# Moving a fused kernel's weights and matmul operands to 512-byte boundaries of the on-chip memory

## The chip, the cores and the metric

The kernel runs on one core of a Trainium2 chip. The metric is the device time of one execution in microseconds (us). Times of the kernel before come from three runs; the rows further down come from one profiled execution.

## What is computed

Three stages, one after the other, all in float32 (reference cut to its core):

```python
X = fft(fft(x, axis=1), axis=2).real                 # x: 4 x 3072 x 256
xk = mu_k * X + (1 - mu_k) * X_prev                  # X_prev: X moved by one token
xr = mu_r * X + (1 - mu_r) * X_prev
k = maximum(xk @ w_k, 0)                             # 256 x 1024
x3 = sigmoid(xr @ w_r) * ((k * k) @ w_v)             # 256 x 256, 1024 x 256
# a mixture of 8 experts over the 12288 rows of x3: expert = argmax of x3 @ w_gate,
# each expert takes its first 384 rows, in order of the tokens
h = maximum(rows_of_expert @ w1[e], 0)
out[row] = probability * (h @ w2[e])                 # rows that no expert took stay 0
```

## The kernel before

The program is written out by engine, with a semaphore for each hand-over; nothing in it orders work by cost, and every address in the on-chip memory is fixed when it is built.

The Fourier transform of a batch is three steps of small matmuls (step1, L1301; step2, L1316; step3, L1328). The middle stage then goes over tiles of 512 tokens (TOK), six to a batch. For a tile, VectorE forms the two mixes (`difference`, `mix`), ScalarE and VectorE split each mix into a high part and a low part (`xk[:, 0]`, `xk[:, 1]`, and `xr` alike), and TensorE multiplies. Every float32 product is made of three matmuls in the faster float32 format (fp32r): high x high, high x low, low x high (`product`, L303). A tile has 8 `up` products of 6 matmuls (weights `wk`, moving operand `xk`), 8 `down` steps of 6 (weights `wv`, moving `k2`) and 12 matmuls for the gate (weights `wr`, moving `xr`). All of them move 512 columns, except 16 of the very first tile that move halves of 256 (`opening_ups`, L1434). Between `up` and `down` stand, for each f, ScalarE's relu (L776) and its copy of the square's high part (L771), and VectorE's square (L1102) and low part (L1097). The Fourier steps of the next batch are put between the products of tiles 3 to 5 of a batch.

After each tile its rows are routed to the experts. When all eight are full, which with these inputs is after 14 tiles, every engine leaves the loop. The expert stage uses other buffers: `xe` (moving, 384 columns, weights `up0_high`, `up0_low`, `up1`) and `down_w` (moving, 256 columns, weights `he`), again three fp32r matmuls to a product.

Addresses: `sb(...)` reserves a buffer of the on-chip memory. The buffers lie one behind the other in the order of the calls, each at the next multiple of 32 bytes (of the bytes of one partition, the same in all 128). A buffer in a `with ExitStack()` of its own gives its place back, so that the next one lies over it: `k2` lies over `raw_wk`, `raw_wr`, `first_partner`, `between` and `raw_wv`. `ph(...)` (L141) reserves what only the Fourier and the middle stage use; `phase1.close()` (L433) gives all of it back, and the expert stage's buffers begin at the same place.

From the sizes in the code: the first `ph` buffer begins at byte 54,784, which is 107 x 512. Then come `c_first` with 6,760 bytes, `c_second` with 1,032 and `c_third` with 960. They and their padding take 8,800 bytes, or 17 x 512 + 96, so `wk`, `wv` and `wr` all begin 96 bytes past a multiple of 512. Behind `wr` come buffers of odd sizes up to `xt`, and `xr_raw`, `xk_raw`, `xk`, `xr`, `relu`, `square`, the `k2` group, `gate_r` and `x3` all begin 224 bytes past one. Both remainders are multiples of 32 and not of 64. In the expert stage `xe`, `raw_up_0`, `raw_up_1`, `raw_down1`, `up1`, `down_w0`, `down_w1` and `he` begin at multiples of 512, and so do `up0_low` and `up0_high`.

Of the kernel before, what the change touches and what calls it, by code (L numbers as in the profile page):

```python
# [18 lines left out]
P = 128  # L19
BATCH, SEQ, DIM, FF = 4, 3072, 256, 1024  # L20
# [5 lines left out]
SETS = FOLDED + 1  # L26
# [14 lines left out]
DH = DIM // P  # L41
FT = FF // P
TOK = 512
# [9 lines left out]
K2S = 8  # L53
# [42 lines left out]
def build(nc, ins, out, cap):  # L96
    fp32, bf16, fp32r = mybir.dt.float32, mybir.dt.bfloat16, mybir.dt.float32r
# [13 lines left out]
    def sb(name, shape, dt=fp32, where=ctx):  # L111
        return where.enter_context(nc.sbuf_tensor(name, shape, dt))
# [26 lines left out]


    ph = lambda name, shape, dt=fp32: sb(name, shape, dt, phase1)  # L141
    c_first = ph("c_first_sb", [P, NR, 2 * JOWN])
    c_second = ph("c_second_sb", [P, ZW])
    c_third = ph("c_third_sb", [P, C3_COLS])
    m_even, m_odd = c_third[0:ROWS2, 0:SCOLS], c_third[0:ROWS2, SCOLS:2 * SCOLS]

    wk = ph("wk", [P, 2, DH, FF], fp32r)
    wv = ph("wv", [P, 2, FT, DIM], fp32r)
    wr = ph("wr", [P, 2, DH, DIM], fp32r)
    fan = ph("fan", [P, DH, SPLIT])  # L150
    mu_k = ph("mu_k", [P, DH])
    mu_r = ph("mu_r", [P, DH])
# [8 lines left out]
    odd_copy = ph("odd_copy", [P, 2, 4 * SCOLS])  # L161
    later_partner = y[:, :, :, :].rearrange("p o q r -> p (o q r)")[:, 0:SETS * DIM].rearrange("p (a d) -> p a d", a=SETS)
    xt = ph("xt", [P, DH, SEQ + 2])
    xr_raw = ph("xr_raw", [P, DH, TOK])
    xk_raw = ph("xk_raw", [P, DH, TOK])
    xk = ph("xk", [P, 2, DH, TOK], fp32r)
    xr = ph("xr", [P, 2, DH, TOK], fp32r)

    relu = ph("relu", [P, 2, TOK])
    square = ph("square", [P, 2, TOK])  # L170
    with ExitStack() as before_k2:
        raw_wk = sb("raw_wk", [P, DH, FF], fp32, before_k2)
        raw_wr = sb("raw_wr", [P, DH, DIM], fp32, before_k2)
        first_partner = sb("first_partner", [P, SETS, DIM], fp32, before_k2)
        sb("between", [P, 2 * K2S * TOK - DH * FF - DH * DIM - FT * DIM - SETS * DIM], fp32, before_k2)
        raw_wv = sb("raw_wv", [P, FT, DIM], fp32, before_k2)
    k2 = ph("k2", [P, 2, K2S, TOK], fp32r)
    gate_r = ph("gate_r", [P, DH, TOK])
    x3 = ph("x3", [P, DH, TOK])
    blank = ph("blank", [P, ROW])  # L180
    least = ph("least", [P, NTILE + 2], i32)
    base = ph("base", [P, EXPERTS])
# [1502 lines left out]
```

## Time and profile before

| | |
|---|---|
| median of 3 runs | 606.15 us (605.74 to 606.67) |
| the profiled execution's own time | 605.92 us |
| its span, first to last instruction | 604.1 us |
| TensorE (PE) busy | 592.7 us, 98% |
| weight loads (PEld) busy | 512.9 us, 85% |
| VectorE (DVE) busy | 449.2 us, 74% |
| ScalarE (ACT) busy | 319.7 us, 53% |
| GpSimd (POOL) busy | 97.5 us, 16% |

How to read it: matmuls run in a pipeline, so that one is still under way when the next begins. The duration of one (some 396 ns for 512 columns) is therefore not what it costs in a dense row of them. What it costs is the time from one start to the next, which is the start of a run of matmuls taken from the start of what follows it, divided by their count. Or the busy time of a run less the duration of its last matmul, divided by one less than their count.

### The profile page before, as it was taken

How to read it: one execution, taken by the hardware profiler on the slowest of the kernel's cores; microseconds unless marked ns; L12 is line 12 of the kernel's file. 1: busy time of each engine (PE TensorE's matmuls, PEld its weight loads, DVE VectorE, ACT ScalarE, POOL GpSimd, SP SyncE). 2: the span in 40 equal slices, each digit the busy share in tenths (PEclk: the TensorE clock that was granted, in tenths of full speed). 3: DMA queues.
4: the chain of work that ended last, by engine and by line, in shares of the span. 5: the costliest groups of instructions: out<-in, count | busy, mean ns of one | idle time of the engine just before them, and what ended most of it. 6: DMA issues, size and time to landing. Idle time of an engine off the chain costs nothing.

```text
span 604.1 us, 9905 instructions
## 1 busy us (share of the span) xinstructions
PE 592.7 (98%) x3356; PEld 512.9 (85%) x3356; DVE 449.2 (74%) x1046; ACT 319.7 (53%) x731; POOL 97.5 (16%) x101
## 2 busy tenths in 40 slices
PE   8999999999999999999999999999998999999996
PEld 4978788888888888888888888888887999999996
DVE  4688888877777688888777776688886777766672
ACT  1674645554546564645454536564647555664450
POOL 0710302020202010202020202011202111011111
PEclk9999999999999999999999999999999999999999
DMA  9429936241510005201010100024003944455100
GB/s 310 153 73 215 395 138 204 94 142 53 185 52 24 2 11 187 105 0 57 10 38 1 34 1 5 30 67 173 32 0 105 365 158 135 160 194 179 41 28 27
DMA packets 42168, 63.14 MB, mean 105 GB/s; under 512 B 4582, under 2 KB 32055, under 8 KB 42108
## 3 DMA queue, kind: packets, MB, share of 16 engines
q1 hardware_dynamic: 38268, 55.88, 28.5%
q0 software_dynamic: 3840, 6.52, 3.1%
q8 instruction: 30, 0.49, 0.3%
q14 instruction: 30, 0.25, 0.1%
HBM read 39.90 MB, written 26.91 MB: 111 GB/s over the span
## 4 chain that ended last, share of the span: by engine, by line
PE 93%; DVE 1%; ACT 1%; SPq 1%; DMA 1%; issue 1%; POOLq 0%; ACTq 0%; DVEq 0%
PE bank L303 71%; PE bank L1407 6%; PE bank L1372 4%; PE bank L1316 3%; PE bank L1328 2%; PE bank L1301 2%; DMA first_partner<-in_x 1%; PE bank L1599 1%; PE bank L1420 1%; DVE xt L958 0%; SPq L485 0%; SPq L496 0%; PE bank L1608 0%; PE bank L1609 0%; PE bank L1612 0%
## 5 line engine op out<-in xcount | busy, mean ns | idle before, releaser
L303 PE MATMUL bank<-k,wv 128*128 128x512 f32 x672 | 165.3, 396 | 0.0
L303 PEld LDWEIGHTS bank<-k,wv 128*128 128x128 f32 x672 | 125.7, 188 | 28.8
L303 PE MATMUL bank<-xk,wk 128*128 128x512 f32 x492 | 124.0, 398 | 0.0
L645 POOL DMA_INDIRECT dispatched<-rows,slot x56 | 60.8, 1086 | 361.2 <-DVE slot L1073 348.4
L303 PEld LDWEIGHTS bank<-xk,wk 128*128 128x128 f32 x492 | 91.3, 189 | 20.0
L776 ACT ACTIVATE relu<-bank 128x512 f32<-128x512 f32 x114 | 67.8, 598 | 74.6 <-PE bank L303 63.1
L1102 DVE TENSOR_TENSOR square<-relu 128x512 f32<-128x512 f32 x113 | 77.9, 691 | 35.0 <-ACT relu L776 31.5
L1097 DVE TENSOR_TENSOR k<-square,k 128x512 fp32r<-128x512 f32 x112 | 76.9, 687 | 2.8 <-ACT k L771 2.8
L771 ACT ACTIVATE k<-square 128x512 fp32r<-128x512 f32 x113 | 70.7, 626 | 11.5 <-DVE square L1102 11.4
L303 PE MATMUL bank<-down_w,he 128*128 128x256 f32 x576 | 72.0, 284 | 0.0
L303 PEld LDWEIGHTS bank<-down_w,he 128*128 128x128 f32 x576 | 70.4, 191 | 0.0
L1267 DVE SCALAR_TENSOR_TENSOR he<-bank,he 128x384 fp32r<-128x384 f32 x64 | 35.7, 558 | 35.3 <-ACT he L898 34.9
L898 ACT ACTIVATE he<-bank 128x384 fp32r<-128x384 f32 x64 | 31.5, 492 | 55.8 <-PE bank L303 29.3
L665 POOL DMA_INDIRECT out_rows<-ye,who x24 | 23.4, 973 | 116.4 <-DVE ye L1281 95.4
L1407 PE MATMUL bank<-xk,wk 128*128 128x512 f32 x144 | 41.2, 409 | 0.0
L303 PE MATMUL bank<-xr,wr 128*128 128x512 f32 x162 | 40.1, 396 | 0.0
L303 PEld LDWEIGHTS bank<-xr,wr 128*128 128x128 f32 x162 | 30.4, 188 | 6.9
L1116 DVE TENSOR_TENSOR x<-gate_r,bank 128x512 f32<-128x512 f32 x28 | 19.1, 687 | 18.6 <-PE bank L303 18.5
L757 ACT ACTIVATE rows<-bank 128x16 f32<-128x16 f32 x56 | 9.5, 184 | 42.6 <-PE bank L1372 41.4
L751 ACT ACTIVATE xr<-xr_raw 128x512 fp32r<-128x512 f32 x30 | 19.0, 633 | 24.4 <-DVE xr_raw L969 24.0
L303 PE MATMUL bank<-xe,up_high 128*128 128x384 f32 x112 | 28.5, 335 | 1.6 <-DVE he L1267 1.6
L303 PE MATMUL bank<-xe,up 128*128 128x384 f32 x168 | 29.8, 334 | 0.0
(151 smaller groups left out, 796.4 us busy)
## 6 DMA issues: line engine op xcount, KB each, us to landing
out_rows<-blank SPq DMA_DIRECT2D x16, 768.0 KB, 4.5
raw_up<-in_moe_w SPq DMA_DIRECT2D x8, 1024.0 KB, 5.2
raw_down<-in_moe_w SPq DMA_DIRECT2D x8, 1024.0 KB, 9.0
got<-dispatched SPq DMA_DIRECT2D x16, 409.5 KB, 3.0
x_area<-in_x SPq DMA_DIRECT2D x12, 384.0 KB, 5.8
y<-in_x SPq DMA_DIRECT2D x9, 384.0 KB, 7.7
dispatched<-blank SPq DMA_DIRECT2D x1, 3276.0 KB, 19.6
first_partner<-in_x SPq DMA_DIRECT2D x3, 384.0 KB, 6.3
```

Of the source, the lines that this page charges most:

```text
L303: done = nc.tensor.matmul(bank, w, x, start=first and i == 0, stop=last and i == len(terms) - 1)
L645: nc.gpsimd.indirect_dma_start(out=slots_dram, out_offset=bass.IndirectOffsetOnAxis(ap=slot[:, g:g + 1], axis=0), in_=rows[:, g, :], in_of ...
L665: nc.gpsimd.indirect_dma_start(out=out, out_offset=bass.IndirectOffsetOnAxis(ap=who[:, i, j:j + 1], axis=0), in_=ye[:, i, j, :], in_offset ...
L771: nc.scalar.activation(k2_at(0, f), square[:, f % 2, :], ACT.Copy).then_inc(k2_high, 1)
L776: nc.scalar.activation(relu[:, f % 2, :], up_bank(n, f)[:, :], ACT.Relu).then_inc(hb_drained, 1)
L898: nc.scalar.activation(he[:, 0, f, :], hbe[f % 3][:, 0:cap], ACT.Relu).then_inc(he_high, 1)
L1097: nc.vector.tensor_tensor(k2_at(1, f), square[:, f % 2, :], k2_at(0, f).bitcast(fp32), ALU.subtract).then_inc(squared, 1)
L1102: nc.vector.tensor_tensor(square[:, f % 2, :], relu[:, f % 2, :], relu[:, f % 2, :], ALU.mult).then_inc(square_ready, 1)
L1116: nc.vector.tensor_tensor(x3[:, h, :], gate_r[:, h, :], vb[h][:, :], ALU.mult).then_inc(x3_done, 1)
L1267: nc.vector.scalar_tensor_tensor(he[:, 1, f, :], hbe[f % 3][:, 0:cap], 0.0, he[:, 0, f, :].bitcast(fp32), ALU.max, ALU.subtract).then_inc( ...
L1372: done = mm(tb[g][:, h * SPLIT:(h + 1) * SPLIT], x3[:, h, g * P:(g + 1) * P], fan[:, h, :], start=True, stop=True)
L1407: done = mm(hb[f % 2][:, :], *terms[k], start=k == 0, stop=k == len(terms) - 1)
```

## The change

The order of the calls to `ph` is changed, and nothing else. `wk`, `wv`, `wr`, `xr_raw`, `xk_raw`, `xk`, `xr`, `relu`, `square`, the group under `k2`, `k2`, `gate_r` and `x3` are reserved first. Their sizes are all multiples of 512 bytes, so each begins at a multiple of 512. `c_first`, `c_second`, `c_third` and the other buffers follow. The moved buffers take 110,592 bytes together, or 216 x 512, which is how far the three constants move up; everything from `fan` to `xt` moves up by 73,728, or 144 x 512. So these keep their remainders by 512. From `blank` on, and in the expert stage, every address is what it was. No instruction, wait, transfer or size changes.

```diff
     ph = lambda name, shape, dt=fp32: sb(name, shape, dt, phase1)
+    wk = ph("wk", [P, 2, DH, FF], fp32r)
+    wv = ph("wv", [P, 2, FT, DIM], fp32r)
+    wr = ph("wr", [P, 2, DH, DIM], fp32r)
+    xr_raw = ph("xr_raw", [P, DH, TOK])
+    xk_raw = ph("xk_raw", [P, DH, TOK])
+    xk = ph("xk", [P, 2, DH, TOK], fp32r)
+    xr = ph("xr", [P, 2, DH, TOK], fp32r)
+    relu = ph("relu", [P, 2, TOK])
+    square = ph("square", [P, 2, TOK])
+    with ExitStack() as before_k2:
+        raw_wk = sb("raw_wk", [P, DH, FF], fp32, before_k2)
+        raw_wr = sb("raw_wr", [P, DH, DIM], fp32, before_k2)
+        first_partner = sb("first_partner", [P, SETS, DIM], fp32, before_k2)
+        sb("between", [P, 2 * K2S * TOK - DH * FF - DH * DIM - FT * DIM - SETS * DIM], fp32, before_k2)
+        raw_wv = sb("raw_wv", [P, FT, DIM], fp32, before_k2)
+    k2 = ph("k2", [P, 2, K2S, TOK], fp32r)
+    gate_r = ph("gate_r", [P, DH, TOK])
+    x3 = ph("x3", [P, DH, TOK])
+
     c_first = ph("c_first_sb", [P, NR, 2 * JOWN])
     c_second = ph("c_second_sb", [P, ZW])
     c_third = ph("c_third_sb", [P, C3_COLS])
     m_even, m_odd = c_third[0:ROWS2, 0:SCOLS], c_third[0:ROWS2, SCOLS:2 * SCOLS]
 
-    wk = ph("wk", [P, 2, DH, FF], fp32r)
-    wv = ph("wv", [P, 2, FT, DIM], fp32r)
-    wr = ph("wr", [P, 2, DH, DIM], fp32r)
     fan = ph("fan", [P, DH, SPLIT])
...
     xt = ph("xt", [P, DH, SEQ + 2])
-    xr_raw = ph("xr_raw", [P, DH, TOK])
...
-    x3 = ph("x3", [P, DH, TOK])
     blank = ph("blank", [P, ROW])
```

## Rows read from the trace of the kernel before

**Rows 1.** The page, busy time and share of the span of each engine.
```profile
PE 592.7 (98%) x3356; PEld 512.9 (85%) x3356; DVE 449.2 (74%) x1046; ACT 319.7 (53%) x731; POOL 97.5 (16%) x101
```
**Rows 2.** Stretch, busy PE, PEld, DVE, ACT, POOL, granted clock, DMA share, GB/s.
```profile
44.00:100.00 56.00, 56.00 (x267) 45.79 (x266) 46.52 (x102) 31.18 (x65) 9.20 (x8) 1.00 0.83 245
100.00:250.00 150.00, 149.74 (x792) 124.78 (x791) 115.14 (x267) 79.91 (x172) 19.32 (x18) 1.00 0.26 89
400.00:455.00 55.00, 55.00 (x266) 44.89 (x265) 44.92 (x109) 29.36 (x64) 8.52 (x8) 1.00 0.22 75
```
**Rows 3.** Whom TensorE waited for, the longest: us in total, times, longest.
```profile
PE bank L385 <- DVE relu L910: 2.0, 1, 2.0
```
**Rows 4.** TensorE's groups, shapes kept apart: count, busy us, mean ns.
```profile
L303 PE MATMUL bank<-k,wv 128*128 128x512 f32 x672 | 165.3, 396 | 0.0
L303 PE MATMUL bank<-xk,wk 128*128 128x512 f32 x492 | 124.0, 398 | 0.0
L1407 PE MATMUL bank<-xk,wk 128*128 128x512 f32 x144 | 41.2, 409 | 0.0
```
**Rows 5.** Timeline of TensorE, middle stage: start us, busy us, what.
```profile
103.84 8.53 PE L303 MATMUL bank<-k,wv 128*128 128x512 f32 x36
112.20 0.63 PE L1407 MATMUL bank<-xk,wk 128*128 128x512 f32 x2
```
**Rows 6.** The critical chain in order of time, two of its pieces.
```profile
8.17 6.61 DMA first_partner<-in_x
62.87 22.31 PE bank L303 x96
```
**Rows 7.** Timeline of TensorE, expert stage.
```profile
512.61 7.44 PE L303 MATMUL bank<-xe,up 128*128 128x384 f32 x42
519.88 3.03 PE L303 MATMUL bank<-down_w,he 128*128 128x256 f32 x24
523.76 5.55 PE L303 MATMUL bank<-down_w,he 128*128 128x256 f32 x45
```
**Rows 8.** Timeline of TensorE, 33.5 to 34.2 us: nine of the opening's half-width matmuls.
```profile
33.22 1.23 PE L1434 MATMUL bank<-xk,wk 128*128 128x256 f32 x9
```
**Rows 9.** Single matmuls by tile: duration ns min/median/max, first and last start.
```profile
L303 PE MATMUL bank<-k,wv x672: 387/393/496, 43.8 to 449.1; 128*128 128x512 f32 x168
L303 PE MATMUL bank<-xe,up x168: 333/334/335, 477.4 to 590.1; 128*128 128x384 f32 x168
L1434 PE MATMUL bank<-xk,wk x16: 279/282/361, 32.5 to 34.4; 128*128 128x256 f32 x16
L303 PE MATMUL bank<-down_w,he x576: 278/283/364, 467.1 to 598.8; 128*128 128x256 f32 x192
```
**Rows 10.** VectorE's and ScalarE's groups: count, busy us, mean ns.
```profile
L1102 DVE TENSOR_TENSOR square<-relu 128x512 f32<-128x512 f32 x113 | 77.9, 691 | 35.0 <-ACT relu L776 31.5
L1267 DVE SCALAR_TENSOR_TENSOR he<-bank,he 128x384 fp32r<-128x384 f32 x64 | 35.7, 558 | 35.3 <-ACT he L898 34.9
L1246 DVE TENSOR_TENSOR down_w<-raw_down,down_w 128x256 fp32r<-128x256 f32 x56 | 19.4, 422 | 0.0
L771 ACT ACTIVATE k<-square 128x512 fp32r<-128x512 f32 x113 | 70.7, 626 | 11.5 <-DVE square L1102 11.4
L885 ACT ACTIVATE down_w<-raw_down 128x256 fp32r<-128x256 f32 x56 | 17.9, 413 | 1.0 <-DMA raw_down<-in_moe_w 1.0
L808 ACT ACTIVATE gate_r<-bank 128x512 f32<-128x512 f32 x28 | 16.6, 598 | 13.6 <-PE bank L303 13.5
L898 ACT ACTIVATE he<-bank 128x384 fp32r<-128x384 f32 x64 | 31.5, 492 | 55.8 <-PE bank L303 29.3 <-PE bank L1612 25.9 <-issue 0.7
```
**Rows 11.** The page, DMA issues: KB each, median us from issue to landing.
```profile
y<-in_x SPq DMA_DIRECT2D x9, 384.0 KB, 7.7
x_area<-in_x SPq DMA_DIRECT2D x12, 384.0 KB, 5.8
first_partner<-in_x SPq DMA_DIRECT2D x3, 384.0 KB, 6.3
```

More of the change, by code:

```diff
@@ L141, in build @@
     ph = lambda name, shape, dt=fp32: sb(name, shape, dt, phase1)
[L142 to L145, printed above, removed]
     wk = ph("wk", [P, 2, DH, FF], fp32r)
@@ L149, in build @@
     wr = ph("wr", [P, 2, DH, DIM], fp32r)
-    fan = ph("fan", [P, DH, SPLIT])
-    mu_k = ph("mu_k", [P, DH])
-    mu_r = ph("mu_r", [P, DH])
-    earlier = ph("earlier", [P, P], bf16)
-    ones = ph("ones", [P, P], bf16)
-    x_area = ph("x_area", [P, max(SETS * DIM, SG * ZW)])
-    x_own = x_area[:, 0:SETS * DIM].rearrange("p (a d) -> p a d", a=SETS)
-    apart = ph("apart", [P, 2])
-    z = x_area[0:ROWS2, 0:SG * ZW].rearrange("p (q k) -> p q k", q=SG)
-    edge = ph("edge", [N2, N1])
-    far_copy = ph("far_copy", [P, 2, 6 * JOWN])
-    odd_copy = ph("odd_copy", [P, 2, 4 * SCOLS])
-    later_partner = y[:, :, :, :].rearrange("p o q r -> p (o q r)")[:, 0:SETS * DIM].rearrange("p (a d) -> p a d", a=SETS)
-    xt = ph("xt", [P, DH, SEQ + 2])
     xr_raw = ph("xr_raw", [P, DH, TOK])
@@ L179, in build @@
     x3 = ph("x3", [P, DH, TOK])
+    c_first = ph("c_first_sb", [P, NR, 2 * JOWN])
+    c_second = ph("c_second_sb", [P, ZW])
+    c_third = ph("c_third_sb", [P, C3_COLS])
+    m_even, m_odd = c_third[0:ROWS2, 0:SCOLS], c_third[0:ROWS2, SCOLS:2 * SCOLS]
+    fan = ph("fan", [P, DH, SPLIT])
+    mu_k = ph("mu_k", [P, DH])
+    mu_r = ph("mu_r", [P, DH])
+    earlier = ph("earlier", [P, P], bf16)
+    ones = ph("ones", [P, P], bf16)
+    x_area = ph("x_area", [P, max(SETS * DIM, SG * ZW)])
+    x_own = x_area[:, 0:SETS * DIM].rearrange("p (a d) -> p a d", a=SETS)
+    apart = ph("apart", [P, 2])
+    z = x_area[0:ROWS2, 0:SG * ZW].rearrange("p (q k) -> p q k", q=SG)
+    edge = ph("edge", [N2, N1])
+    far_copy = ph("far_copy", [P, 2, 6 * JOWN])
+    odd_copy = ph("odd_copy", [P, 2, 4 * SCOLS])
+    later_partner = y[:, :, :, :].rearrange("p o q r -> p (o q r)")[:, 0:SETS * DIM].rearrange("p (a d) -> p a d", a=SETS)
+    xt = ph("xt", [P, DH, SEQ + 2])
     blank = ph("blank", [P, ROW])
```

## The prediction

> **What bounds the kernel now.** I read the engines' busy time first [rows 1]. TensorE is busy 98% of the span, VectorE 74%, so if an address changes anything it has to change TensorE to matter. Then the stretches [rows 2]: through the middle stage TensorE is busy without a gap (56.00 of 56.00 us, 149.74 of 150.00, 55.00 of 55.00), at the full granted clock, that is 2.4 GHz or 0.417 ns for a column. VectorE has 83% there (46.52 of 56.00), 77% (115.14 of 150.00) and 82% (44.92 of 55.00). TensorE's longest wait on anyone in the whole span is 2.0 us, once, at the start [rows 3]. So a matmul of the middle stage that takes less time gives nearly all of it to the end, and one that takes more costs all of it.
>
> The quantity that decides is the time from one matmul's start to the next one's. Three widths of fp32r matmul are there, each with its own remainder of the address by 512:
>
> - 512 columns, middle stage, weights 96 and moving operand 224 bytes past a boundary: 36 matmuls from 103.84 to 112.20 us, or 8.36 / 36 = 232.2 ns [rows 5]. A second stretch: 96 in 22.31 us, or 232.4 ns [rows 6]. I take 232.3.
> - 384 columns, expert stage, everything at multiples of 512: 42 from 512.61 to 519.88 us, 7.27 / 42 = 173.1 ns; by the busy time, (7.44 - 0.334) / 41 = 173.3 ns [rows 7, 9]. I take 173.3.
> - 256 columns, expert stage, at multiples of 512: (5.55 - 0.283) / 44 = 119.7 ns [rows 7, 9].
> - 256 columns, the opening of the first tile, off the boundary as the 512-wide ones are: (1.23 - 0.282) / 8 = 118.5 ns [rows 8, 9].
>
> **The change part by part.** It removes, adds and moves no instruction; only addresses differ. There are four kinds of operation whose address changes.
>
> *Fp32r matmuls of 512 columns.* Their number: 672 + 492 + 144 in the three largest groups [rows 4] and 214 in eight smaller ones, 1,522 in all. The code gives the same: 14 tiles of 48 + 48 + 12, less the 8 that the opening moves as 16 halves, and 18 of a fifteenth tile that are issued ahead of leaving the loop. Their cost at a boundary is not in the trace, so it is bounded from the aligned rows. Lower end: from 256 to 384 columns the aligned start-to-start time grows by 173.3 - 119.7 = 53.6 ns, and 128 columns at 0.417 ns are 53.3. So in the aligned stage width costs the clock alone and all else is constant (173.3 - 384 x 0.417 = 13.3 ns). One more step of 128 columns gives 173.3 + 53.3 = 226.6 ns, where the row shows 232.3: the unaligned matmul has 5.7 ns that the aligned rule doesn't explain. Upper end, if the 13.3 ns grow with width: 173.3 x 512 / 384 = 231.1 ns, 1.2 below today. Both start from the same nearest row, and nothing in the trace puts the truth nearer to either, so I take the middle, 228.85 ns, 3.45 ns less than now. 1,522 x 3.45 ns = 5.25 us, and the ends are 1,522 x 1.2 = 1.8 us and 1,522 x 5.7 = 8.7 us.
>
> A second sign that the address does something: the durations of the single aligned matmuls of 384 columns agree to 2 ns (333/334/335). Those of the 512-wide ones have 393 for a median but mean 396 [rows 4, 9], and the minimum is 387.
>
> *VectorE and ScalarE on the moved buffers.* VectorE takes 422 ns for 256 columns and 558 for 384, both on the boundary, and 691 for 512 off it: the step that crosses over costs 133 ns, the one that stays costs 136. ScalarE: from 256 columns on the boundary to 512 off it (source in the same memory, 413 and 626 ns) are 213 ns, and from 384 on to 512 off it (source in the accumulation banks, 492 and 598 ns) are 106 [rows 10]. With a rate r a column and a cost c of being off, 256 r + c = 213 and 128 r + c = 106, so that c is -1 ns. I take 0. Even 10 ns on each of the some 500 large operations of VectorE would lie under TensorE's busy time, since VectorE has 17% to spare; were that cover gone, it would cost 5 us.
>
> *Small matmuls* (Fourier steps, routing): `c_first`, `c_second`, `c_third`, `x_area`, `fan` and `y` keep their remainders. Only `x3` as weights moves. 0, within 0.2 us.
>
> *Transfers.* `first_partner`, `raw_wk`, `raw_wr` and `raw_wv` now land on boundaries. One matters: 6.61 us of `first_partner` stand in the chain that ends last [rows 6]. Transfers of 384 KB took 5.8 us into `x_area`, 6.3 into `first_partner` (both 224 past a boundary) and 7.7 into `y` (480 past one) [rows 11], so their spread is the queue's, not the address's. I take 0, bounds -0.4 and +0.4 us.
>
> The sum: 605.92 us is the profiled execution's own time (span 604.1 and 1.8 around it). 605.92 - 5.25 = 600.7. That execution lies 0.23 us under the median of the runs, which puts the forecast at 600.9 us. As TensorE gets 1.5% faster VectorE's share there goes from 83% to 84%; no new bound arises, though the places where VectorE is the later one give back a little, perhaps 0.1 us: 601.0.
>
> **The rivals.**
>
> *The address changes nothing that can be measured* (606.15 us; within 0.2%, or 1.2 us, about what a measurement can tell from no change). For it: the one width seen on and off the boundary, 256 columns, doesn't gain on it (119.7 against 118.5 ns). The 5.7 ns may then belong to the width of 512 itself, the only one here that fills a whole accumulation bank. Against it: it leaves an increment of 53.3 ns per 128 columns up to 384 and 59 behind it unexplained but by that. The Trainium skill speaks for this rival: "SBUF — State Buffer", in the note on cachelines under "Door 1: The DMA port swizzle", has lines of 16 bytes as the only grain that an engine's reads feel. All the old remainders are multiples of 32, so by that rule every operand already starts on a line, and the sum would be 605.9.
>
> *On the boundary the matmuls settle into a slower beat* (slower than before). The aligned rows are 119.7 and 173.3 ns, near 18 and 26 times 6.67 ns, with hardly any scatter, while the unaligned 256-wide ones came out at 118.5, between steps. If start times on the boundary lock to such steps, 512 columns may lock at 34 (226.7 ns, the lower end above), but also at 35, which is 233.3 ns. The price of the latter is 1.0 ns x 1,522 = 1.5 us, 607.7 us; the 256-wide pair shows the same sign and size (119.7 - 118.5 = 1.2 ns, 1.8 us if it held for all). At 36 steps, 240 ns, it would be 7.7 ns x 1,522 = 11.7 us, 617.9. It decides against the change from a start-to-start time of 233.1 ns on, where the loss passes 1.2 us. Against it: three steps over the 32 of the columns, where both aligned rows have two.
>
> *The lower end holds in full*: 605.92 - 8.7 + 0.23 = 597.5 us. It is part of the forecast's own range.
>
> **How the numbers follow.** The forecast, faster, the matmuls of 512 columns between 226.6 and 231.1 ns: 0.47, own range 597.2 to 604.6. No change: 0.35. A slower beat at 35 steps: 0.14; at 36 or worse: 0.04. The range goes from 597.0, where the lower end of the matmuls meets 0.4 us from the transfers, to 608.2, which takes in the 35 steps with the same 0.4. It leaves out the 36 steps and a gain beyond the aligned rule. Faster by over 0.2% is the forecast's 0.47, within it 0.35, slower 0.18.
>
> **What would show it.** In the timeline of the changed kernel the run of 36 matmuls of `k` and `wv` after 100 us: 228.85 ns each is 8.24 us to the next start where 8.36 stood; 8.16 is the lower end, 8.40 the slower beat. The widths of 384 and 256 in the expert stage must stay at 173.3 and 119.7, since their addresses don't move; if they change, the cause isn't the address. VectorE's 691 and ScalarE's 598 ns must stay. If TensorE's busy time in the middle stage falls below its full share, VectorE has become a bound and part of the gain is lost. The opening's nine half-width matmuls tell on or off the boundary at one width: toward 119.7 ns the address acts on them. The prediction is wrong if 512 columns keep 232.3 ns, or if they slow down.

## The result: 1.1% faster, and the middle stage's matmuls start every 226.7 ns

The changed kernel takes 599.12 us (median, 598.74 to 600.78) against 605.97 us for the kernel before in the same comparison: a ratio of 0.9888, 95% interval 0.9874 to 0.9902. Its profiled execution took 599.07 us with a span of 597.2, 6.9 us less than the 604.1 of before. The forecast was 601.0 us, within 597.0 to 608.2.

The page of the changed kernel, busy time by engine and then the two largest groups of matmuls (count, busy us, mean ns):

```profile
PE 585.8 (98%) x3356; PEld 511.7 (86%) x3356; DVE 448.8 (75%) x1046; ACT 319.4 (53%) x731; POOL 96.6 (16%) x101
...
L303 PE MATMUL bank<-k,wv 128*128 128x512 f32 x672 | 162.0, 391 | 0.0
...
L303 PE MATMUL bank<-xk,wk 128*128 128x512 f32 x492 | 121.6, 393 | 0.0
```

TensorE's busy time fell by 592.7 - 585.8 = 6.9 us [rows 1], the whole gain. Of it 165.3 - 162.0 = 3.3 us are the 672 matmuls of `k2` and `wv`, and 124.0 - 121.6 = 2.4 us the 492 of `xk` and `wk` [rows 4]. Some 0.2 us have nothing to do with the change: they are the plain float32 matmuls at the opening (L385), both of whose operands lie in `relu`, so that their distance did not change. They went from 9.5 to 9.3 us, and among the experiments they take anything from 9.0 to 10.6. VectorE's 448.8 us and ScalarE's 319.4 are within 0.4 us of what they were.

The timeline of TensorE in the changed kernel (start us, busy us, what), the run of 36 that stands in [rows 5], and the expert stage as in [rows 7]:

```profile
102.28 8.32 PE L303 MATMUL bank<-k,wv 128*128 128x512 f32 x36
110.44 0.62 PE L1407 MATMUL bank<-xk,wk 128*128 128x512 f32 x2
...
505.75 7.44 PE L303 MATMUL bank<-xe,up 128*128 128x384 f32 x42
513.03 3.03 PE L303 MATMUL bank<-down_w,he 128*128 128x256 f32 x24
```

From 102.28 to 110.44 are 8.16 us for 36, or 226.7 ns from start to start where 232.2 stood. The expert stage, whose addresses did not move, has the same 7.44 and 3.03 us as before. The waits of TensorE name nobody new, and the middle stage is still full: busy 56.00 of 56.00 us from 44 to 100, at a granted clock of 1.00, with VectorE's share at 85% where it was 83% [rows 2]:

```profile
44.00:100.00 56.00, 56.00 (x271) 46.55 (x270) 47.59 (x103) 31.20 (x66) 8.99 (x8) 1.00 0.85 252
```

### The profile page after: what moved, and what is told of

Read it like the earlier page. It is cut to its first block, busy times and chain, and to the rows that moved or that the text cites. A ratio compares the mean times of both kernels' runs of the same rounds, so it can differ in the third digit from the quotient of the medians.

```text
span 597.2 us, 9905 instructions
## 1 busy us (share of the span) xinstructions
PE 585.8 (98%) x3356; PEld 511.7 (86%) x3356; DVE 448.8 (75%) x1046; ACT 319.4 (53%) x731; POOL 96.6 (16%) x101
## 4 chain that ended last, share of the span: by engine, by line
PE 93%; DVE 2%; issue 2%; SPq 1%; DMA 1%; ACT 1%; POOLq 0%; DVEq 0%; ACTq 0%
PE bank L303 71%; PE bank L1407 6%; PE bank L1372 4%; PE bank L1316 3%; PE bank L1328 2%; PE bank L1301 2%; DMA first_partner<-in_x 1%; PE bank L1599 1%; PE bank L1420 1%; DVE xt L958 0%; SPq L496 0%; SPq L485 0%; PE bank L1608 0%; PE bank L1609 0%; PE bank L1612 0%
## 5 line engine op out<-in xcount | busy, mean ns | idle before, releaser
L303 PE MATMUL bank<-k,wv 128*128 128x512 f32 x672 | 162.0, 391 | 0.0
L303 PE MATMUL bank<-xk,wk 128*128 128x512 f32 x492 | 121.6, 393 | 0.0
L771 ACT ACTIVATE k<-square 128x512 fp32r<-128x512 f32 x113 | 70.7, 626 | 13.8 <-DVE square L1102 13.4
L898 ACT ACTIVATE he<-bank 128x384 fp32r<-128x384 f32 x64 | 31.5, 492 | 55.9 <-PE bank L303 28.6
L1407 PE MATMUL bank<-xk,wk 128*128 128x512 f32 x144 | 40.9, 406 | 0.0
L303 PEld LDWEIGHTS bank<-xr,wr 128*128 128x128 f32 x162 | 30.3, 188 | 6.4
L303 PE MATMUL bank<-xe,up_high 128*128 128x384 f32 x112 | 28.5, 335 | 1.7 <-issue 1.7
L303 PE MATMUL bank<-xe,up 128*128 128x384 f32 x168 | 29.8, 334 | 0.0
```

The lines of the kernel that those rows point to most:

```text
L303: done = nc.tensor.matmul(bank, w, x, start=first and i == 0, stop=last and i == len(terms) - 1)
L771: nc.scalar.activation(k2_at(0, f), square[:, f % 2, :], ACT.Copy).then_inc(k2_high, 1)
L898: nc.scalar.activation(he[:, 0, f, :], hbe[f % 3][:, 0:cap], ACT.Relu).then_inc(he_high, 1)
L1407: done = mm(hb[f % 2][:, :], *terms[k], start=k == 0, stop=k == len(terms) - 1)
```

## The experiments

What is open after this: whether the gain comes from the boundary (a start at a multiple of 64 or of 512), from the order and place of the buffers, or from something that the new order brings along. The fillers in the edits below keep the buffers that are not named at their old remainders by 512. Three runs are exceptions: in the run with the old order and in the one with a single filler the small buffers from `blank` on move too, and with 32 bytes ahead of `he` so do `prob` and what lies behind it. None of these is an operand of an fp32r matmul.

### All moved buffers 32 or 64 bytes past the boundary

```diff
+    ph("shift", [P, 8])        # 16 in the second run
     wk = ph("wk", [P, 2, DH, FF], fp32r)
...
     x3 = ph("x3", [P, DH, TOK])
+    ph("rest", [P, 120])       # 112 in the second run
```

> The order of the changed kernel, but 32 bytes are reserved ahead of the weights and 480 behind x3, so that every moved buffer lies 32 bytes past a multiple of 512; the others keep their remainders by 512 and move up by 512. Theory (what counts is where the operands lie against a line of 64 bytes): the 512-column matmuls go back to 232.3 ns from start to start where the changed kernel has 226.7, and the time to 606. Rival (what counts is where in the memory the buffers lie, or their order, and the remainder is nothing): 226.7 ns and 599.

> As the run with 32 bytes, but with 64 ahead of the weights and 448 behind x3. Theory with a grain of 64 bytes: nothing is lost, 226.7 ns and 599. Rival with a coarser grain (128, 256 or 512 bytes): 232.3 ns and 606.

Measured: 598.86 us (ratio 0.9879, 0.9851 to 0.9908) with 32 bytes, and 599.49 (0.989, 0.9861 to 0.9918) with 64. The run of 36 in the timeline, 32 bytes:

```profile
102.60 8.32 PE L305 MATMUL bank<-k,wv 128*128 128x512 f32 x36
110.76 0.62 PE L1409 MATMUL bank<-xk,wk 128*128 128x512 f32 x2
```

8.16 us again, 226.7 ns. With all operands 32 bytes off the boundary nothing is lost. My theory, and the title of the change, name the wrong thing: the boundary is not what counts.

What the experiments need is only the distance between buffers, which follows from their sizes. The remainders themselves hang on byte 54,784 for the first `ph` buffer, and that number is not from the sizes in the code alone: those ahead of it come to 46,464, and no trace shows an address. With a start of 46,464 no moved buffer would lie on a multiple of 512, and every conclusion here would be the same.

### Only the weights, or only the moving operands, 32 bytes off

```diff
+    ph("shift", [P, 8])        # ahead of wk, weights alone
     wk = ph("wk", [P, 2, DH, FF], fp32r)
     wv = ph("wv", [P, 2, FT, DIM], fp32r)
     wr = ph("wr", [P, 2, DH, DIM], fp32r)
+    ph("rest", [P, 120])
```

The other run has the 8 columns behind `wr` and the 120 behind `x3`.

> Only wk, wv and wr lie 32 bytes past a multiple of 512; the moving operands xk, xr and k2, and all else, as in the changed kernel (480 bytes are reserved behind wr). If the moving operand alone decides, since it is read at full rate: 226.7 ns and 599. If the weight load decides: 232.3 ns and 606. If both matter: between the two, near 229.5 ns and 602.5.

> The counterpart: wk, wv and wr at multiples of 512, and xr_raw, xk_raw, xk, xr, relu, square, k2, gate_r and x3 lie 32 bytes past one. If the moving operand decides: 232.3 ns and 606. If the weight load decides: 226.7 ns and 599. If both matter: near 229.5 ns and 602.5. If only the place of one against the other matters (in the run with all at 32 the two have the same remainder), this and the run with the weights at 32 are both at 232.3 and the run with all at 32 is at 226.7.

Measured: 606.5 us (ratio 1.0, 0.9988 to 1.0011) with the weights moved, 606.95 (1.0014, 1.0003 to 1.0025) with the moving operands. Timelines, weights moved first, then the moving operands:

```profile
103.90 8.56 PE L305 MATMUL bank<-k,wv 128*128 128x512 f32 x36
112.30 0.63 PE L1409 MATMUL bank<-xk,wk 128*128 128x512 f32 x2
```

```profile
104.38 8.56 PE L305 MATMUL bank<-k,wv 128*128 128x512 f32 x36
112.78 0.63 PE L1409 MATMUL bank<-xk,wk 128*128 128x512 f32 x2
```

Both are 8.40 / 36 = 233.3 ns, though one operand of each pair lies on the boundary. Together with the run before, that is the last case of the second expectation: what counts is the remainder of the weights against that of the moving operand. (The values aren't a fixed step in the single starts: in these two runs the 36 are 230 to 236 ns apart, with 233.3 for a mean.) In the kernel before these were 96 and 224, 128 bytes apart; the change made them equal.

### The old order with equal remainders, and the grain of the difference

```diff
+    ph("to_weights", [P, 104])
     wk = ph("wk", [P, 2, DH, FF], fp32r)
...
     wr = ph("wr", [P, 2, DH, DIM], fp32r)
+    ph("to_fan", [P, 24])
...
+    ph("to_operands", [P, 72])
     xr_raw = ph("xr_raw", [P, DH, TOK])
```

> The old order of the buffers, with 416 bytes reserved ahead of wk, 96 behind wr and 288 ahead of xr_raw: weights and moving operands both at multiples of 512, each within 1 KB of its old place; x_area, fan and the others keep their remainders. The runs before this one showed 226.7 ns with weights and moving operands at the same remainder (0, 32 or 64) and 233 with only one of them moved by 32. Theory (only the difference of the two remainders counts): 226.7 ns and 599. Rival (the order and the place in the memory carry the gain): 232.3 ns and 606.

The next two have the changed kernel's order, with 64 (16) columns of filler behind `wr` and 64 (112) behind `x3`.

> The changed kernel with 256 bytes reserved between wr and xr_raw and 256 behind x3: weights at a remainder of 0, moving operands at 256. Since slices of the weights lie at all multiples of 512, a difference can only count by 512 or a part of it. If its grain is 256: 226.7 ns and 599. If it is 512: near 232 to 233 ns and 606.

> The changed kernel with 64 bytes between wr and xr_raw and 448 behind x3: moving operands 64 bytes off the weights. If lines of 64 bytes are the grain, 226.7 ns and 599. The kernel before, whose difference is 128, had 232.3 ns, so a grain of 64 or 128 is excluded unless its cause is another: I expect 232 to 233.5 ns and 606.

Measured: old order 598.88 us (0.9869, 0.9834 to 0.9904); 256 apart 598.58 (0.9864, 0.9829 to 0.9899); 64 apart 601.85 (0.9926, 0.9904 to 0.9949). Timelines, in this order:

```profile
102.44 8.32 PE L306 MATMUL bank<-k,wv 128*128 128x512 f32 x36
110.60 0.62 PE L1410 MATMUL bank<-xk,wk 128*128 128x512 f32 x2
```

```profile
101.84 8.32 PE L305 MATMUL bank<-k,wv 128*128 128x512 f32 x36
110.00 0.61 PE L1409 MATMUL bank<-xk,wk 128*128 128x512 f32 x2
```

```profile
103.07 8.40 PE L305 MATMUL bank<-k,wv 128*128 128x512 f32 x36
111.31 0.62 PE L1409 MATMUL bank<-xk,wk 128*128 128x512 f32 x2
```

Order and place are excluded: the old order gives 8.16 us for 36 as well. A difference of 256 is as good as none. One of 64 gives 8.24 / 36 = 228.9 ns, between the two, so for 64 my expectation of at least 232 ns and 606 us was a miss; the price isn't all or nothing.

### The kernel before with one filler, and one pair alone

```diff
+    ph("shift", [P, 32])
     xr_raw = ph("xr_raw", [P, DH, TOK])
```

> The kernel before with one edit: 128 bytes reserved ahead of xr_raw. The weights stay 96 bytes past a multiple of 512, x_area and all Fourier buffers keep their very addresses, and xr_raw to x3 move from 224 to 352 bytes past one, so that the difference from weights to moving operand goes from 128 to 256 and nothing of it lies at a multiple of 64. Theory (the difference, by 256, is all that counts): 226.7 ns, 599. Rival (a multiple of 64 is needed on one side at least, or the changed kernel's order): 232.3 ns and 606.

Measured: 599.26 us, ratio 0.9883 (0.9868 to 0.9898), the changed kernel's gain from 128 bytes of filler:

```profile
102.43 8.32 PE L304 MATMUL bank<-k,wv 128*128 128x512 f32 x36
110.59 0.61 PE L1408 MATMUL bank<-xk,wk 128*128 128x512 f32 x2
```

How far the effect reaches, in the changed kernel, with only the weights `wv` moved:

```diff
+    ph("shift", [P, 8])
     wv = ph("wv", [P, 2, FT, DIM], fp32r)
+    ph("rest", [P, 120])
```

> The changed kernel with 32 bytes reserved ahead of wv and 480 behind it, so that only the weights of the down product lie off their moving operand k2; wk with xk and wr with xr stay at the same remainder. Theory (the difference acts on the matmuls whose own weights and moving operand differ, as many times as there are such matmuls): the 672 of k and wv take 233.2 ns, 5.8 more than in the changed kernel, the others keep some 227.9; 672 x 5.8 = 3.9 us, 603.0. Rival (what counts is the layout as a whole, such as all operands of the middle stage at one remainder): all of the 1,522 go to 233 ns, 606.5, or none does, 599.1.

Measured: 603.12 us, ratio 0.995 (0.9933 to 0.9966), against an expected 603.0. The groups of that kernel:

```profile
L305 PE MATMUL bank<-k,wv 128*128 128x512 f32 x672 | 165.7, 397 | 0.0
L305 PE MATMUL bank<-xk,wk 128*128 128x512 f32 x492 | 122.0, 394 | 0.0
```

The `wv` group went back up from 162.0 to 165.7 us, the `wk` group stayed near its 121.6. The effect belongs to each matmul's own pair of operands, and not to the layout as a whole.

### The expert stage: other widths, other best difference

The opening's 256-column matmuls gave the lead: with one side moved by 32 bytes the last nine of the 16 start 118 ns apart on average (weights moved) and 116 (moving operands), where the 256-column ones of [rows 7] have 119.7. Three runs try that in the expert stage. The first puts 8 columns of filler ahead of `he` (weights), the second 8 ahead of `xe` and 8 ahead of `down_w0` with 120 behind each, the third only:

```diff
+    sb("shift_down", [P, 8])
     down_w = [sb(f"down_w{i}", [P, 2, FT, DIM], fp32r) for i in range(2)]
+    sb("rest_down", [P, 120])
```

> The changed kernel with 32 bytes reserved ahead of he, so that in the expert stage's second product the weights (he) lie 32 bytes off the moving operand down_w (256 columns), and nothing else differs. In the two runs with one side moved by 32, the opening's 256-column matmuls took 117 to 118 ns where 119.7 is the value at the same remainder. Theory (at 256 columns the same remainder costs time that it saves at 512): 117.5 ns for the 576 matmuls, 1.3 us less, 597.8. Rival (the same remainder is the faster one at every width): above 120 ns, and over 599.5.

> The changed kernel with the expert stage's moving operands, xe and down_w, 32 bytes past a multiple of 512 and their weights on one (32 bytes reserved ahead of each, 480 behind). Theory (the difference acts on all fp32r matmuls, and its best value depends on the width): down_w's 576 of 256 columns go from 119.7 to 117 ns as the opening's did with the moving side moved, 1.6 us less; the 384-column ones change too, up from 173.3 by some 2 ns if they behave like 512 (0.8 us more), down if like 256. Rival (the expert stage is unlike the middle one and keeps 119.7 and 173.3).

> The changed kernel with only down_w0 and down_w1 32 bytes past a multiple of 512, all else as in the changed kernel: the version that puts each width at the difference that was best for it so far. 256 columns at 117 ns in place of 119.7: 576 x 2.7 ns is 1.6 us, so 597.5 against 599.1 for the changed kernel. Rival (VectorE or ScalarE take over in the expert stage, and the matmuls only wait longer): 599.

Measured: `he` off 598.51 us (0.9863, 0.9825 to 0.99); `xe` and `down_w` off 598.12 (0.9865, 0.9847 to 0.9883); `down_w` alone off 597.24 (0.9849, 0.9836 to 0.9863; five runs, 596.63 to 597.45). Groups, with `he` off (and its timeline), then `xe` and `down_w` off:

```profile
L303 PE MATMUL bank<-down_w,he 128*128 128x256 f32 x576 | 71.1, 282 | 0.0
...
512.57 3.00 PE L303 MATMUL bank<-down_w,he 128*128 128x256 f32 x24
515.41 0.82 PE L1600 MATMUL bank<-small,got 128*128 128x128 f32 x6
```

```profile
L303 PE MATMUL bank<-down_w,he 128*128 128x256 f32 x576 | 70.7, 280 | 0.0
...
L303 PE MATMUL bank<-xe,up 128*128 128x384 f32 x168 | 30.3, 339 | 0.0
L303 PE MATMUL bank<-xe,up_high 128*128 128x384 f32 x112 | 28.6, 336 | 1.7 <-issue 1.7
```

and with `down_w` alone off, group and timeline:

```profile
L303 PE MATMUL bank<-down_w,he 128*128 128x256 f32 x576 | 70.3, 280 | 0.0
...
504.70 7.44 PE L303 MATMUL bank<-xe,up 128*128 128x384 f32 x42
511.98 2.97 PE L303 MATMUL bank<-down_w,he 128*128 128x256 f32 x24
514.79 0.82 PE L1601 MATMUL bank<-small,got 128*128 128x128 f32 x6
```

With the moving side 32 bytes off, 24 matmuls take 514.79 - 511.98 = 2.81 us, 117.1 ns each, and the group falls from 72.0 us, its value in the kernel before and the changed one, to 70.3. With the weights' side off it falls only to 71.1, and the 24 take 515.41 - 512.57 = 2.84 us, 118.3 ns each, so 32 bytes one way are not 32 the other way at this width. The offset between `down_w` and `he` does not settle it alone, either: with `xe` moved as well it is the same, and the group stands at 70.7. Why that run has 0.4 us more was not tested. The rival that equal remainders are best at every width is out. At 384 columns the odd experts (`up`) lose, 29.8 to 30.3 us, and the even ones (`up_high`) are at 28.6 against 28.5, though the remainders are the same in both. Why the two differ was not tested. So the difference of the two remainders, which decides at 512 columns in all runs, is not shown to be the whole rule at the other widths.

The last version beats both kernels by a little: 597.24 us, a ratio to the kernel before whose interval ends at 0.9863, below the 0.9874 at which the changed kernel's begins. The two were not timed in one comparison. Its gain over the changed kernel, 599.12 - 597.24 = 1.9 us, is near the 1.7 us by which its `down_w` group fell.

## Why the prediction was right, and where it wasn't

**The frame held.** TensorE is the bound, its start-to-start time decides, and a gain per matmul reaches the end: 6.9 us of its busy time and 6.85 us of the profiled executions' times. VectorE took nothing back: TensorE's busy time from 44 to 100 us is still the full 56.00, so the 0.1 us that I set aside for it was not needed.

**The mechanism was wrong, and that its number held was in part luck.** I took the remainder of each operand by 512 for the cause. Both stages differ by that, but they also differ by the remainder of the weights against that of the moving operand: 128 bytes apart in the middle stage, 0 in the expert stage. My lower end was "what the aligned stage shows, one step of 128 columns on", and since the change brought the middle stage to the expert stage's difference, 226.6 ns was met to 0.1. It was luck that bringing everything to one boundary also brings the two operands to one remainder; with the weights at 0 and the moving operands at 32 bytes past, one side on the boundary, the same reasoning would have left room for a gain, and that run had none (606.95 us). The step of the prediction that failed is the sentence that lists each width "with its own remainder": it had 96 and 224 in front of it and compared neither with the other.

**The middle between the ends was a mis-sized term.** I took 3.45 ns a matmul, midway between 1.2 and 5.7, on the ground that nothing put the truth nearer to either. The steady run shows 232.2 - 226.7 = 5.5 ns. That ground did not hold: the prediction's own rows leave 119.7 - 256 x 0.417 = 13.0 ns beside the columns at 256 and 13.3 at 384, which is a constant. Growth with the width, as the upper end has it, would ask for 8.9 at 256. The rows spoke for the lower end. (A small slip besides: 607.7 + 0.4 is 608.1, not 608.2; nothing hangs on it.)

**And the lower end was not reached in full, which the sum hid.** It would have been 8.7 us; 6.9 came, 6.7 of them from the matmuls whose operands moved. The sum multiplied one price by 1,522, and the price holds only for a matmul in a long run of its kind. Sorted by how many 512-column fp32r matmuls have passed since the last matmul of another kind, the starts in the two traces give, before and after:

| place behind the interruption | matmuls | start to start, us in all | gain of one |
|---|---|---|---|
| 1 to 4 | 228 | 57.6 and 57.4 | 1.0 ns |
| 5 to 10 | 308 | 72.3 and 71.2 | 3.4 ns |
| 11 and on | 986 | 230.1 and 224.7 | 5.5 ns |

The five other runs with a difference of 0 or 256 bytes in the middle stage alone agree with the changed kernel on the last line, 227.8 or 227.9 ns for one; the two with one side 32 bytes off have 234.1. So the forecast's 5.25 us for the matmuls came near the measured 6.7 by two errors against each other: a price too low by 2 ns for most of them, and a count that took in 536 which gain less or nothing. The timeline behind the routing's small matmuls, changed kernel first, then the kernel before:

```profile
112.66 2.10 PE L1407 MATMUL bank<-xk,wk 128*128 128x512 f32 x8
114.62 0.18 PE L1383 MATMUL bank<-padded,earlier 128*128 128x40 bf16 x1
...
115.29 2.90 PE L303 MATMUL bank<-xr,wr 128*128 128x512 f32 x12
118.03 4.25 PE L303 MATMUL bank<-xk,wk 128*128 128x512 f32 x18
122.12 1.06 PE L1301 MATMUL bank<-c_first_sb,x_area 128*128 128x130 f32 x8
```

```profile
114.43 2.10 PE L1407 MATMUL bank<-xk,wk 128*128 128x512 f32 x8
116.40 0.18 PE L1383 MATMUL bank<-padded,earlier 128*128 128x40 bf16 x1
...
117.07 2.96 PE L303 MATMUL bank<-xr,wr 128*128 128x512 f32 x12
119.87 4.34 PE L303 MATMUL bank<-xk,wk 128*128 128x512 f32 x18
124.05 1.17 PE L1301 MATMUL bank<-c_first_sb,x_area 128*128 128x130 f32 x9
```

In the single stretch that shows it the first 8 take 1.96 us in the one and 1.97 in the other: no gain. The next 12 take 2.74 us, 228.3 ns, against 2.80, 233.3. The 18 behind them take 4.09 us, 227.2 ns, against 4.18, 232.2. So in these traces about ten matmuls pass after other work before the gain is full. The group L1407, of which 120 of 144 stand in the first eight places, shows it: 41.2 us before [rows 4], 40.9 after, 2 ns a matmul.

**The rivals.** "The address changes nothing" had its strongest argument in the one width seen both ways, 256 columns, which was not faster on the boundary. That observation was right and not an argument: at 256 columns an unequal remainder is the faster one, at 512 the equal one, as the expert stage's runs showed. The rule that stood beside that rival is that of the Trainium skill, "SBUF — State Buffer", the note on cachelines under "Door 1: The DMA port swizzle": accesses that stay in a line of 16 bytes run at full bandwidth. The note speaks of one stream of accesses and names no larger grain. It is not contradicted for an operand alone, as all operands moved by 32 together cost nothing; but 5.5 ns hang on the two operands' relation. The same page, under "Who interferes with whom", gives TensorE two independent read ports, one for the moving operand and one for the weight load. By that the relation of the two addresses should do nothing; the runs at 226.7 and 233.3 ns differ in it alone, and the measurement decides. The slower beat at 35 steps of 6.67 ns, 233.3 ns, did not come in the changed kernel. The other half of that rival did: in the run of 36 the single starts, which lay 228 to 241 ns apart before, are all 226 or 227 ns apart now, at 34 of those steps. That the means with either operand moved by 32 bytes come out at 35 steps is no sign of a lock, since their single starts scatter from 230 to 236.

**The opening's sign came too.** At one width and in one place, nine of the half-width matmuls before [rows 8] have 118.5 ns; in the changed kernel, from the window 33.4 to 34.1 us:

```profile
33.12 1.24 PE L1434 MATMUL bank<-xk,wk 128*128 128x256 f32 x9
```

(1.24 - 0.283) / 8 = 119.6 ns, and the last nine starts of the 16 are 120 ns apart each. The prediction had this as the sign that the address acts on them. It is 1 ns slower, as the expert stage's 256-column runs then confirmed.

**The small terms.** VectorE and ScalarE: 0 was right within 2 ns, 690 ns for the square where 691 stood, and 600 for `gate_r` where 598 did [rows 10]. The transfer of `first_partner` in the chain went from 6.61 [rows 6] to 6.13 us in one execution, yet the opening's first matmul starts at 32.34 us instead of 32.55, so 0.2 us at most come from there, inside the bounds given. Among the experiments with a difference of 0 or 256 bytes that start lies anywhere from 31.91 to 32.71 us, so it is scatter as far as the runs tell.

## What to carry to other kernels

When TensorE is dense and its matmuls load new weights each time, look at the addresses of its two operands together: compare (address of the weights) - (address of the moving operand) by 256, and try it at 0 for wide matmuls before anything is rewritten. It costs a filler of at most a few hundred bytes. Measure each width for itself, by the start-to-start time in a long run of the timeline and not by the mean duration of one matmul, and don't read a shared property of two stages as the cause while a relation between their operands would fit as well.

## What the hardware showed that was not expected

- Fp32r matmuls of 512 columns with their own weights each, start to start, by the difference of the remainders: 0 and 256 bytes 226.7 ns; 64 bytes (moving operand ahead) 228.9; 128 bytes 232.2; 32 bytes, either way, 233.3. Each is read from a run of 36 in one execution, at a granted clock of 1.00 from 101 to 111 us in every one of these runs. Other differences were not tried.
- Of 256 columns: equal 119.7 ns; weights 32 bytes past the moving operand 118.3; moving operand 32 bytes past the weights 117.1.
- A change of the address reaches the first four matmuls after other work by 1.0 ns each, and those from the eleventh on by 5.5.
- Why the difference counts is open. That the weight load and the moving read get in each other's way in the memory is a guess; no run here looks into it, and it is not shown.
